# One attention kernel's first forty microseconds: the first pair's key rows sent in halves ahead of the second pair's key loads, and the second pair's turning moved into the first score slots

## The chip, the cores and the metric

The kernel runs on one core of one Trainium2 chip. The metric is device microseconds (us) of one execution; a time quoted without more is the median of several runs. Lower is better.

## The reference

The inputs are `q`, `k`, `v` of shape (2, 8, 768, 64), a projection of shape (64, 6), and the weights of two expert layers. Only the first part matters here:

```python
q_bits = (np.einsum('bhsd,dk->bhsk', q, proj) > 0)
k_bits = (np.einsum('bhsd,dk->bhsk', k, proj) > 0)
q_bucket, k_bucket = np.sum(q_bits * powers, -1), np.sum(k_bits * powers, -1)
mask = q_bucket[:, :, :, None] == k_bucket[:, :, None, :]
scores = np.where(mask, scale * q @ k.T, -1e9)      # per head
attn = exp(scores - max); attn /= sum(attn) + 1e-9
attn_out = attn @ v
x = moe(attn_out)      # dense: h = x w_in, a rational function of h, times w_out
out = moe2(x)          # each token to the expert with the largest logit
```

A query may only see keys whose six projection signs equal its own. Sixteen heads of 768 rows go through this, then 1536 tokens through a dense layer and through eight experts.

## The kernel before

Heads are taken in eight **pairs**; the two heads of a pair lie side by side in the 128 partitions (64 channels each). Each float32 matrix is split into a rounded high part and a rest (`qk_hi`, `qk_lo`), so that matmuls of rounded operands keep the precision. For each head an **operand** tile of four planes is built. Plane 0 and plane 1 are the stationary side of the score matmuls (high and low query rows; high query rows and query mask words). Plane 2 and plane 3 are the moving side (key rows twice; low key rows and key mask words). Two matmuls per bank then give score plus mask penalty at once.

**Preparing a pair** takes ten steps, `step(p, k)`, with one PSUM bank (number 7) between them. Steps 0 to 3 turn the loaded rows: three transposes on TensorE (PE), and an eviction to `raw` by ScalarE (ACT, steps 0 and 2, queries) or VectorE (DVE, steps 1 and 3, keys). GpSimd (POOL) then splits each half into `qk_hi` and `qk_lo` (`split_qk`). Steps 4 and 7 are six projection matmuls whose signs ACT writes to `bits`; steps 5, 6, 8 and 9 are one matmul each, whose mask words DVE writes. Each step waits until the one before it has been evicted. Rows that must change partition go by DMA from SyncE's queue (SP): `operand_rows`, `mask_rows`.

**The first pair** has a faster path of its own. It is loaded in halves of three tiles, turned into banks 0 to 3, and split straight out of PSUM by ACT (`first_split`: `qk_hi`) and DVE (`qk_lo`). PE projects the halves (`first_proj_hi`, `first_proj_lo`), ACT takes the signs, PE multiplies by `sel` (`first_sel`), and DVE (`first_mask`) and ACT (`first_word`) write the mask words. POOL copies the rows of head 0 that stay in their partitions (`first_own`), and SP sends the rows that change partition.

**The order of work** is written out by hand, in slots numbered `s`. Every second slot starts a score tile `scores(g)` (4 matmuls, `g = s/2`), which waits for `exp_done >= g - 1`, since two score tiles share the banks. DVE takes the row maximum (`maxs`), ACT the exponential (`exps`). From slot 7 PE turns the exponentials in chunks (`turn(c)`), ACT and DVE split them (`hi(c)`, `lo(c)`), and from slot 10 PE multiplies them by the values (`pv(j)`). `PREP_AT_1` names the slots after which the ten steps of the second pair stand: 3, 6, 7, 8, 9, ... 14. The third pair's first step is at slot 15. `keep_warm(n, bank)` is n matmuls of 512 columns on zeros, to no use but to keep PE going: 9 before the first load has landed, 3 ahead of slot 0, and 3 in each of slots 3, 4 and 6.

**SP's queue** at the start: the identity, the first pair's queries, two blocks of constants, then head 0 of the second pair (queries and keys), the first half of the low query rows (after `first_lo` 1), the second head's queries, the key rows of both halves in one transfer (after `first_hi` 4), the second half of the low query rows (after `first_lo` 3), the second head's keys, the values, and the rows of head 1.

Of the kernel before, what the change touches and what calls it, by code (L numbers as in the profile page):

```python
# [15 lines left out]
P = 128  # L16
B, H, S, D = 2, 8, 768, 64
NBITS = 6
# [97 lines left out]
def build(nc, q, k, v, proj, w_in, w_out, a, b, w_gate, w1, w2, consts, out):  # L116
    ctx = ExitStack()
    M4 = QF // P
    with ctx:
# [189 lines left out]
        s_half = sem("s_half")  # L309
        s_qk = [sem(f"s_qk{i}") for i in range(2)]  # L310
        s_v = [sem(f"s_v{i}") for i in range(2)]
        s_op = [[sem(f"s_op{i}{o}") for o in range(2)] for i in range(2)]
# [136 lines left out]
        PREP_AT = [1, 2, 3, 4, 8, 9, 10, 12, 13, 14]  # L449
        PREP_AT_1 = [3, 6, 7, 8, 9, 10, 11, 12, 13, 14]  # L450
        PREP_AHEAD = 10
# [69 lines left out]
        def op_landed(p, o):  # L521

            return 96 * (p // 2 + 1) - (0 if p % 2 else (64, 16)[o])

# [39 lines left out]
        def _(sp):  # L564
# [66 lines left out]
            sp.dma_start(cst[:, P:C_END], consts[:, P:C_END]).then_inc(s_const, 16)  # L631
            load_qk_head(1, 0, 0)
            load_qk_head(1, 0, 1)
            sp.wait_ge(first_lo, 1)
            sp.dma_start(operands[0][0][D:P, 0, 0:HALF].bitcast(F32), qk_lo[0][0:D, 0, 0:HALF].bitcast(F32)).then_inc(s_op[0][0], 16)
            load_qk_head(1, 1, 0)
            sp.wait_ge(first_hi, 4)
            sp.dma_start(operands[0][0][D:P, 2, :].bitcast(F32), qk_hi[0][0:D, 1, :].bitcast(F32)).then_inc(s_op[0][0], 16)
            sp.wait_ge(first_lo, 3)
            sp.dma_start(operands[0][0][D:P, 0, HALF:S].bitcast(F32), qk_lo[0][0:D, 0, HALF:S].bitcast(F32)).then_inc(s_late_lo, 16)  # L640
            load_qk_head(1, 1, 1)
            load_v(0)
# [83 lines left out]
        def _(pool):  # L726
# [52 lines left out]
            pool.wait_ge(first_lo, 4)  # L779
            pool.tensor_copy(operands[0][0][0:D, 3, :], qk_lo[0][0:D, 1, :].bitcast(F32)).then_inc(first_own, 1)  # L780
            split_v(0)
            split_qk(1, 0)
            split_qk(1, 1)
# [92 lines left out]
        def _(act):  # L876
# [9 lines left out]

            act.wait_ge(s_proj, 32)
            act.wait_ge(zeroed, 2)
            for x in range(4):
                rows = slice(x % 2 * D, (x % 2 + 1) * D)  # L890
                act.activation(wproj[rows, x // 2 * 2, x * NBITS:(x + 1) * NBITS], pr_raw[rows, :], ACT.Copy).then_inc(proj_hi, 1)
            first_split(0)
# [8 lines left out]
            def first_word(half, o):  # L901
# [4 lines left out]
                               scale=BIG, bias=cst[other, C_CUT:C_CUT + 1]).then_inc(first_high, 1)  # L906

            first_word(1, 0)
            first_word(0, 1)
            first_word(1, 1)  # L910
# [222 lines left out]
        def _(dve):  # L1133
# [5 lines left out]
            def first_split(half):  # L1139

                for x in range(2):
                    k, c = 2 * half + x, slice(half * HALF, (half + 1) * HALF)
                    dve.wait_ge(first_hi, k + 1)
                    dve.scalar_tensor_tensor(out=qk_lo[0][:, x, c], in0=ps[:, k, 0:HALF], scalar=(0.125, 1.0)[x], in1=qk_hi[0][:, x, c].bitcast(F32), op0=ALU.mult, op1=ALU.subtract).then_inc(first_lo, 1)

            dve.wait_ge(proj_hi, 4)
            for x in range(4):
# [21 lines left out]
            def step(p, k):  # L1169
# [5 lines left out]
                if k in (1, 3):  # L1175
                    dve.wait_ge(prep_pe, m + 1)
                    if k == 1 and p >= 2:
                        for o in range(2):
                            dve.wait_ge(s_op[p % 2][o], op_landed(p - 2, o))
                    dve.tensor_copy(raw[p % 2][:, 1, c], bank).then_inc(prep_out, 1)  # L1180
                elif k in (5, 8):
                    dve.wait_ge(prep_pe, m + 1)
                    if k == 5:
                        for o in range(2):
                            dve.wait_ge(s_op[(p - 1) % 2][o], op_landed(p - 1, o))
                    dve.tensor_scalar(mask[:, 0, c], bank, NBITS - 0.5, BIG, ALU.is_ge, ALU.mult).then_inc(prep_out, 1)
                elif k in (6, 9):
                    dve.wait_ge(prep_pe, m + 1)
                    dve.tensor_scalar(mask[:, 1, c], bank, -float(NBITS), -1.0, ALU.add, ALU.max).then_inc(prep_out, 1)
# [280 lines left out]
        def _(pe):  # L1470
            def step(p, k):
# [6 lines left out]
                if m == 0:  # L1478
                    pe.wait_ge(first_dve, 1)
                    pe.wait_ge(first_high, 2)  # L1480
                if k < 4:
                    pe.wait_ge(s_qk[p % 2], 64 * (p // 2 + 1))
                    for t in range(HT):
# [23 lines left out]
            def scores(g):  # L1507
# [4 lines left out]
                if g == 0:  # L1512
                    pe.wait_ge(first_own, 3)
                    pe.wait_ge(first_dve, 3)
                    pe.wait_ge(first_high, 1)
                if g == HT:
                    pe.wait_ge(s_late_lo, 16)
                if g == NT:
                    pe.wait_ge(first_dve, 5)
                    pe.wait_ge(first_high, 3)  # L1520
# [95 lines left out]
            first_sel(1)  # L1616
            keep_warm(3, 3)

            for s in range(NSLOT):
# [15 lines left out]
                if prep_at(s):  # L1635
                    step(*prep_at(s))
                if s == 3:
                    pe.wait_ge(first_dve, 4)
                if s in (3, 4, 6):
                    keep_warm(3, 6)  # L1640
                r = turn_r_at(s)
# [328 lines left out]
```

## Time and profile before

| | us |
|---|---|
| median of 3 runs | 802.01 (801.35 to 804.67) |
| profiled execution, its own time | 802.68 |
| profiled execution, span from first to last instruction | 800.8 |
| PE busy in the span | 782.6 |
| DVE, ACT, POOL busy | 563.2, 498.6, 457.8 |

Busy time counts work, not the issue of DMAs. PE's busy time includes the matmuls on zeros, and the modelled end of a matmul overlaps the next one, so the distance between two starts is the better price of a matmul than its duration. PE is the LDWEIGHTS and MATMUL engine; PEld is its weight load alone; SPq is SyncE's queue issuing a DMA.

### The profile page before, as it was taken

The page shows a single profiled execution, that of the slowest core. Times are in us where ns is not written, and L with a number is a line of the kernel's source. Part 1 is how long each engine was busy: PE and PEld are TensorE (multiplying, and loading weights), DVE is VectorE, ACT ScalarE, POOL GpSimd, SP SyncE. Part 2 cuts the span into 40 slices and gives each one's busy share as a digit, 9 for nine tenths or more (in the row PEclk, how much of TensorE's full clock was granted, in tenths as well). Part 3 has the DMA queues.
Part 4 walks back from the last instruction along what each step waited for, and adds up shares of the span by engine and source line. Part 5 has one row for each costly group of instructions (what it writes and reads, how often), then busy time and mean ns, then how long its engine had stood idle before and what let it go on. Part 6 is the DMA issues. An engine that isn't in the chain of part 4 may idle for free.

```text
span 800.8 us, 13465 instructions
## 1 busy us (share of the span) xinstructions
PE 782.6 (98%) x4305; PEld 692.0 (86%) x4305; DVE 563.2 (70%) x973; ACT 498.6 (62%) x988; POOL 457.8 (57%) x405
## 2 busy tenths in 40 slices
PE   8899999999999999999999999999899999999997
PEld 6799899899998989999999999997688888888886
DVE  5788888888887787887778877997354454444542
ACT  5688878878898998778778877874332224222100
POOL 3425265265257687457647744533997659755810
PEclk9999999999999999999999999997999999999999
DMA  8899977985841760950692041063664447433200
GB/s 194 171 215 199 211 164 168 204 169 132 191 150 53 237 244 0 338 203 1 204 374 83 1 156 55 3 206 125 210 234 151 181 146 254 155 132 132 68 33 19
DMA packets 71986, 123.49 MB, mean 154 GB/s; under 512 B 33358, under 2 KB 36270, under 8 KB 67824
## 3 DMA queue, kind: packets, MB, share of 16 engines
q1 hardware_dynamic: 64320, 90.77, 41.9%
q10 hardware_dynamic: 5056, 25.56, 8.9%
q0 software_dynamic: 2544, 6.31, 2.2%
q8 instruction: 37, 0.61, 0.3%
q14 instruction: 29, 0.24, 0.1%
HBM read 60.33 MB, written 34.24 MB: 118 GB/s over the span
## 4 chain that ended last, share of the span: by engine, by line
PE 90%; ACT 3%; issue 2%; DVE 2%; DMA 1%; POOL 0%; POOLq 0%; SPq 0%; ACTq 0%; DVEq 0%
PE ps L1538 7%; PE ps L1574 6%; PE ps L1576 6%; PE ps L1575 6%; PE ps L1675 5%; PE ps L1676 5%; PE ps L1674 5%; PE ps L1872 4%; PE ps L1904 4%; PE ps L1902 4%; PE ps L1903 4%; PE ps L1873 4%; PE ps L1877 4%; PE ps L1525 4%; PE ps L1550 4%; PE ps L1526 4%
## 5 line engine op out<-in xcount | busy, mean ns | idle before, releaser
L841 POOL TENSOR_TENSOR split<-wraw,split 128x512 f32 (+1 forms) x112 | 140.5, 1296 | 46.3 <-ACT split L1031 42.1
L1031 ACT ACTIVATE split<-wraw 128x512 f32 (+1 forms) x128 | 69.4, 619 | 120.3 <-PE ps L1904 56.2
L1215 DVE TENSOR_TENSOR ptl<-ps,pth 128x512 fp32r<-128x512 f32 x144 | 98.8, 686 | 37.2 <-ACT pth L945 35.3
L945 ACT ACTIVATE pth<-ps 128x512 fp32r<-128x512 f32 x144 | 86.5, 601 | 32.9 <-PE ps L1538 32.8
L816 POOL TENSOR_TENSOR hw<-hw,ha 128x384 f32<-128x384 f32 x64 | 65.3, 1020 | 72.3 <-ACT hw L981 72.3
L1195 DVE TENSOR_REDUCE negmax<-ps 128x1 f32<-128x768 f32 x96 | 91.0, 949 | 8.5 <-PE ps L1526 8.5
L936 ACT ACTIVATE pr<-ps,negmax 128x768 f32<-128x768 f32 x96 | 86.8, 904 | 4.2 <-DVE negmax L1195 4.2
L1538 PE MATMUL ps<-cst,pr 128*128 128x128 f32 x576 | 88.0, 273 | 1.2 <-ACT pr L936 1.2
L1574 PE MATMUL ps<-xh,wih 128*128 128x384 f32 x256 | 86.6, 338 | 0.0
L1576 PE MATMUL ps<-xh,wil 128*128 128x384 f32 x256 | 86.3, 337 | 0.0
L1575 PE MATMUL ps<-xl,wih 128*128 128x384 f32 x256 | 85.9, 336 | 0.0
L551 POOL TENSOR_TENSOR gl<-ha,gh 128x384 fp32r<-128x384 f32 x64 | 65.0, 1016 | 27.7 <-ACT gh L545 27.7
L1538 PEld LDWEIGHTS ps<-cst,pr 128*128 128x128 f32 x576 | 69.8, 140 | 8.6 <-ACT pr L936 2.2
L1550 PE MATMUL ps<-pth,vs 128*128 128x384 f32 x192 | 74.3, 387 | 0.2
L1525 PE MATMUL ps<-operand 128*128 128x384 f32 x192 | 68.8, 358 | 1.2 <-DMA operand<-qk_hi 0.7
L1676 PE MATMUL ps<-woh,gl 128*128 128x512 f32 x168 | 66.5, 396 | 0.0
L1675 PE MATMUL ps<-wol,gh 128*128 128x512 f32 x168 | 66.4, 395 | 0.0
L1674 PE MATMUL ps<-woh,gh 128*128 128x512 f32 x168 | 65.4, 389 | 0.0
L1551 PE MATMUL ps<-ptl,vs 128*128 128x384 f32 x192 | 64.9, 338 | 0.0
L1526 PE MATMUL ps<-operand 128*128 128x384 f32 x192 | 64.6, 337 | 0.0
L1443 DVE TENSOR_SCALAR yo<-ps,gi 128x512 f32<-128x512 f32 x18 | 13.5, 750 | 68.1 <-PE ps L1904 68.1
L1902 PE MATMUL ps<-split,hth 128*128 (+1 forms) x144 | 57.7, 401 | 1.1 <-DVE htl L1434 1.1
(240 smaller groups left out, 2018.7 us busy)
## 6 DMA issues: line engine op xcount, KB each, us to landing
routed<-blank SPq DMA_DIRECT2D x33, 771.0 KB, 13.6
wraw<-in_moe_w ACTq DMA_DIRECT2D x24, 1024.0 KB, 6.5
wraw<-in_moe_w SPq DMA_DIRECT2D x8, 1024.0 KB, 6.2
operand<-qk_hi SPq DMA_DIRECT2D x31, 192.0 KB, 4.6
operand<-qk_hi SPq DMA_DIRECT2D x15, 384.0 KB, 4.9
operand<-qk_lo SPq DMA_DIRECT2D x30, 192.0 KB, 4.3
operand<-mask SPq DMA_DIRECT2D x14, 384.0 KB, 5.2
xg<-routed SPq DMA_DIRECT2D x19, 256.0 KB, 2.7
```

Source lines behind the costliest of these rows:

```text
L841: pool.tensor_tensor(split_piece(E_LO[x], ring, k), wraw[:, x, i, :], split_piece(E_HI[x], ring, k).bitcast(F32), ALU.subtract).then_inc(e ...
L1215: dve.tensor_tensor(ptl[:, at:at + CW], ps[:, 4 + c % 2, :], pth[:, at:at + CW].bitcast(F32), ALU.subtract).then_inc(ptl_done, 1)
L1525: pe.matmul(bank, operand_of(n, 0)[:, rows], operand_of(n, 2)[:, cols], start=True, stop=False)
L1526: mm = pe.matmul(bank, operand_of(n, 1)[:, rows], operand_of(n, 3)[:, cols], start=False, stop=True)
L1538: mm = pe.transpose(ps[:, 4 + c % 2, x * P:(x + 1) * P], pr[u % UNITS][:, t, kt * P:(kt + 1) * P], ident)
L1550: pe.matmul(ps[:, 6, 0:HALF], vs[n % 2][:, kt, :], pth[:, cols], start=(kt == 0), stop=False)
L1574: pe.matmul(bank, wh[:, kt, f], xh[bb][:, kt, cols], start=(kt == 0), stop=False)
L1575: pe.matmul(bank, wh[:, kt, f], xl[bb][:, kt, cols], start=False, stop=False)
L1576: mm = pe.matmul(bank, wl[:, kt, f], xh[bb][:, kt, cols], start=False, stop=(kt == KD - 1))
L1674: pe.matmul(ps[:, 4 + t, :], gh[s % 2][:, m, rows], woh[qq % 2][:, m, :], start=(m == 0), stop=False)
L1675: pe.matmul(ps[:, 4 + t, :], gh[s % 2][:, m, rows], wol[qq % 2][:, m, :], start=False, stop=False)
L1676: mm = pe.matmul(ps[:, 4 + t, :], gl[s % 2][:, m, rows], woh[qq % 2][:, m, :], start=False, stop=(m == M4 - 1))
```

## The change

1. SP loads both heads' queries of the second pair ahead of everything that waits, under a semaphore of their own (`s_second_q`). The key rows of head 0 go in two halves, the first as soon as `first_hi` is 2. Both key loads of the second pair stand behind them, and the second half of the low query rows behind those.
2. The copies that make the high part of `wproj` move from ACT to DVE.
3. ACT's mask words come in another order (head 1's first half first). `scores(0)` no longer waits for `first_high`; `scores(3)` does.
4. Step 0 of the second pair stands ahead of slot 0, the other steps at slots 2, 4, 6, 8, 9, 10, 11, 12 and 13. The matmuls on zeros fall from 3 to 1 ahead of slot 0, and from 9 to 3 inside the slots (2 in slot 2, 1 in slot 6).
5. POOL splits the second pair's first half before it splits head 0's values. The mask step of the second pair no longer waits for head rows of the first.

```diff
-        PREP_AT_1 = [3, 6, 7, 8, 9, 10, 11, 12, 13, 14]
+        PREP_AT_1 = [-1, 2, 4, 6, 8, 9, 10, 11, 12, 13]
...
-            return 96 * (p // 2 + 1) - (0 if p % 2 else (64, 16)[o])
+            return 96 * (p // 2 + 1) - (0 if p % 2 else (48, 16)[o])
...
-            load_qk_head(1, 0, 0)
-            load_qk_head(1, 0, 1)
+            for o in range(2):
+                sp.dma_start(nat[1][:, 0, :, o, :], q_h[2 + o, :, :, :]).then_inc(s_second_q, 16)
+
+            def first_rows(x, plane, rows, half, landed):
+
+                c = slice(half * HALF, (half + 1) * HALF)
+                sp.dma_start(operands[0][0][D:P, plane, c].bitcast(F32), rows[0:D, x, c].bitcast(F32)).then_inc(landed, 16)
+
+            sp.wait_ge(first_hi, 2)
+            first_rows(1, 2, qk_hi[0], 0, s_op[0][0])
             sp.wait_ge(first_lo, 1)
-            sp.dma_start(operands[0][0][D:P, 0, 0:HALF].bitcast(F32), qk_lo[0][0:D, 0, 0:HALF].bitcast(F32)).then_inc(s_op[0][0], 16)
-            load_qk_head(1, 1, 0)
+            first_rows(0, 0, qk_lo[0], 0, s_op[0][0])
             sp.wait_ge(first_hi, 4)
-            sp.dma_start(operands[0][0][D:P, 2, :].bitcast(F32), qk_hi[0][0:D, 1, :].bitcast(F32)).then_inc(s_op[0][0], 16)
+            first_rows(1, 2, qk_hi[0], 1, s_op[0][0])
+            for o in range(2):
+                load_qk_head(1, o, 1)
             sp.wait_ge(first_lo, 3)
-            sp.dma_start(operands[0][0][D:P, 0, HALF:S].bitcast(F32), qk_lo[0][0:D, 0, HALF:S].bitcast(F32)).then_inc(s_late_lo, 16)
-            load_qk_head(1, 1, 1)
+            first_rows(0, 0, qk_lo[0], 1, s_late_lo)
...
+            split_qk(1, 0)
             split_v(0)
-            split_qk(1, 0)
...
-            act.wait_ge(s_proj, 32)
-            act.wait_ge(zeroed, 2)
-            for x in range(4):
-                rows = slice(x % 2 * D, (x % 2 + 1) * D)
-                act.activation(wproj[rows, x // 2 * 2, x * NBITS:(x + 1) * NBITS], pr_raw[rows, :], ACT.Copy).then_inc(proj_hi, 1)
...
+            first_word(0, 1)
             first_word(1, 0)
-            first_word(0, 1)
...
+            dve.wait_ge(s_proj, 32)
+            dve.wait_ge(zeroed, 2)
+            for x in range(4):
+                rows, cols = slice(x % 2 * D, (x % 2 + 1) * D), slice(x * NBITS, (x + 1) * NBITS)
+                dve.tensor_copy(wproj[rows, x // 2 * 2, cols], pr_raw[rows, :]).then_inc(proj_hi, 1)
...
-                    if k == 5:
+                    if k == 5 and p >= 2:
...
-                    pe.wait_ge(first_high, 2)
+                    pe.wait_ge(first_high, 1)
                 if k < 4:
-                    pe.wait_ge(s_qk[p % 2], 64 * (p // 2 + 1))
+                    if p == 1 and k % 2 == 0:
+                        pe.wait_ge(s_second_q, 32)
+                    else:
+                        pe.wait_ge(s_qk[p % 2], 64 * (p // 2 + 1) - (32 if p % 2 else 0))
...
-                    pe.wait_ge(first_high, 1)
                 if g == HT:
                     pe.wait_ge(s_late_lo, 16)
+                    pe.wait_ge(first_high, 2)
...
-            keep_warm(3, 3)
+            step(1, 0)
+            keep_warm(1, 3)
...
-                if s == 3:
+                if s == 2:
                     pe.wait_ge(first_dve, 4)
-                if s in (3, 4, 6):
-                    keep_warm(3, 6)
+                if s in (2, 6):
+                    keep_warm((2, 1)[s // 6], 6)
```

## Rows read from the trace of the kernel before

**Rows 1.** The page: busy time, share of the span and instructions

```profile
PE 782.6 (98%) x4305; PEld 692.0 (86%) x4305; DVE 563.2 (70%) x973; ACT 498.6 (62%) x988; POOL 457.8 (57%) x405
```

**Rows 2.** Windows: from:to, length, busy us of each engine, granted clock, DMA share, GB/s

```profile
8.00:13.00 5.00, 3.93 (x20) 2.65 (x20) 3.96 (x9) 3.76 (x8) 3.00 (x3) 1.00 0.75 163
...
40.00:50.00 10.00, 10.00 (x66) 9.43 (x65) 8.22 (x13) 7.80 (x16) 4.48 (x5) 1.00 0.99 215
```

**Rows 3.** PE's waits from 0 to 60 us: total, times, longest

```profile
PE ps L1489 <- DVE raw L1180: 0.7, 1, 0.7
...
PE ps L1484 <- DVE raw L1180: 0.4, 1, 0.4
```

**Rows 4.** Timeline of the start: start, us, what, idle before and its releaser

```profile
5.48 2.49 PE L1587 MATMUL ps<-cst,nat 128*128 128x128 f32 x12
5.79 0.90 ACT L891 ACTIVATE wproj<-pr_raw 64x6 fp32r<-64x6 f32 x4 [1.55 <-DMA pr_raw<-in_proj]
6.71 1.85 ACT L885 ACTIVATE qk_hi<-ps 128x384 fp32r<-128x384 f32 x4
6.71 0.73 DVE L1149 TENSOR_TENSOR wproj<-pr_raw,wproj 64x6 fp32r<-64x6 f32 x4 [4.60 <-ACT wproj L891]
...
8.56 0.19 PEld L1600 LDWEIGHTS ps<-qk_lo,wproj 128*128 128x128 f32 x1 [0.20 <-DVE qk_lo L1144]
...
10.43 0.82 POOL L780 CAST operand<-qk_lo 64x768 fp32r<-64x768 f32 x1
...
10.92 2.12 DVE L1161 TENSOR_SCALAR operand<-ps 64x384 fp32r<-64x384 f32 x4
11.27 1.65 ACT L905 ACTIVATE operand<-ps,cst 64x384 fp32r<-64x384 f32 x3 [0.43 <-PE ps L1607]
...
12.83 0.44 PE L1525 MATMUL ps<-operand 128*128 128x384 f32 x1 [0.74 <-DMA operand<-qk_hi]
```

**Rows 5.** DMA issues by kind, 0 to 13 us: KB each, us to landing

```profile
operand<-qk_lo SPq DMA_DIRECT2D x2, 96.0 KB, 2.8
operand<-qk_hi SPq DMA_DIRECT2D x1, 192.0 KB, 3.5
```

**Rows 6.** Groups of one shape, 0 to 60 us: busy us, mean ns, idle before

```profile
L1195 DVE TENSOR_REDUCE negmax<-ps 128x1 f32<-128x768 f32 x18 | 17.0, 951 | 5.1 <-PE ps L1526 5.1
L1215 DVE TENSOR_TENSOR ptl<-ps,pth 128x512 fp32r<-128x512 f32 x21 | 14.4, 685 | 6.4 <-ACT pth L945 6.1
...
L936 ACT ACTIVATE pr<-ps,negmax 128x768 f32<-128x768 f32 x17 | 15.3, 901 | 3.0 <-DVE negmax L1195 3.0
L945 ACT ACTIVATE pth<-ps 128x512 fp32r<-128x512 f32 x21 | 12.6, 598 | 8.0 <-PE ps L1538 8.0
...
L735 POOL TENSOR_TENSOR qk_lo<-raw,qk_hi 128x768 fp32r<-128x768 f32 x4 | 7.3, 1834 | 0.3
```

**Rows 7.** The chain that ended last: start, us on the chain, what

```profile
16.91 0.70 PE ps L1556 x3
...
18.31 0.33 PE ps L1484 x3
```

**Rows 8.** Timeline of PE later: start, us, what, idle before

```profile
15.94 0.44 PE L1525 MATMUL ps<-operand 128*128 128x384 f32 x1 [0.43 <-ACT pr L936]
...
27.15 0.41 PE L1525 MATMUL ps<-operand 128*128 128x384 f32 x1
...
33.63 0.55 PE L1484 MATMUL ps<-cst,nat 128*128 128x128 f32 x3 [0.55 <-DVE mask L1189]
...
37.84 0.42 PE L1525 MATMUL ps<-operand 128*128 128x384 f32 x1
```

**Rows 9.** DMA issues by kind, 0 to 40 us

```profile
nat<-in_k SPq DMA_DIRECT2D x4, 192.0 KB, 3.9
```

**Rows 10.** Timeline and windows about 545 us

```profile
543.48 1.91 PE L1699 MATMUL ps<-wg,yt 128*128 128x8 f32 x16
...
545.00:550.00 5.00, 4.79 (x19) 3.59 (x19) 3.86 (x21) 4.14 (x9) 1.60 (x2) 0.68 0.28 86
```

More of the change, by code:

```diff
@@ L310, in build @@
         s_qk = [sem(f"s_qk{i}") for i in range(2)]
+        s_second_q = sem("s_second_q")
         s_v = [sem(f"s_v{i}") for i in range(2)]
```

## The prediction

> **What bounds the kernel now.** I read the page first. PE is busy 782.6 of 800.8 us [rows 1], so only 18.2 us are to be had at all without taking real work from it, and the change takes away no real work: it touches the first forty microseconds and leaves the rest alone. The windows come next. From 40 to 50 us PE is busy for all 10.00 us [rows 2]; from there on what PE has gained earlier it keeps, and it can gain no more. So the question is how much earlier PE reaches that steady stretch. For this I read PE's waits from 0 to 60 us and then the timeline. The reader is to see four waits for the work this change moves: 0.7 us of a projection for an eviction of the second pair and 0.4 us for another eviction [rows 3], 0.74 us for the key rows' transfer ahead of `scores(0)` [rows 4], and 0.55 us of the third pair's first transposes for the last mask words of the second, shown with the later rows. Beside them lie the matmuls on zeros, which count as busy and are none: twelve from slot 0's front to slot 6.
>
> **What the start gains.** `scores(0)` starts at 12.83 us, behind the key rows, which took 3.5 us to land and so left at 9.3 [rows 4, 5]. This is one transfer of 192 KB behind a load of the second pair that was issued just before it.
>
> After the change the first transfer is due when ACT's second `qk_hi` piece is there. ACT loses its four copies to `wproj` (5.79 to 6.69), but PE's transposes run from 5.48 to 7.97, and the last of ACT's four pieces begins at 6.71 + 3 x 1.85 / 4 = 8.1 already, 0.1 behind the last transpose [rows 4]. So the first two pieces come up to 0.3 earlier, the last two at the old time, 8.56. The last half of the key rows is then issued at about 8.7, the queue being free, and its 96 KB land after the 2.8 us of such pieces [rows 5], at 11.5, at the latest after the 3.5 of today's 192 KB, at 12.2.
>
> DVE makes the copies ACT made. The trace has no such copy on DVE; the nearest row is its subtraction of the same shape, 0.73 / 4 = 0.18 each with its gap [rows 4]. As bounds I take that and half of it: the low part of `wproj` is done at 5.79 + 8 x 0.18 = 7.2, or at 6.9. DVE's first `qk_lo` piece can start at 7.2 instead of just after 6.71 + 0.73 = 7.44. PE takes 0.2 of this, its idle time before L1600 [rows 4]; the rest is bound by its own transposes. So the signs, the mask matmuls and the mask words come 0.2 earlier. `scores(0)` waits for the third mask piece of DVE: today 10.92 and two of the four pieces of 2.12, so 12.0 [rows 4], then 11.8. This is the later of the two, and ahead of it PE fits step 0 (three transposes, 0.35, from 11.3, when ACT's first mask word has freed the bank; ACT's words start when `bits` is written, 0.4 ahead of today's 11.27) and one matmul on zeros, to 11.9. POOL's own copies are done at 10.43 + 0.82 = 11.25 [rows 4] and stay so. **`scores(0)` starts at 11.9 instead of 12.83: 0.9 us**, and the cause of waiting is now DVE, no longer a transfer.
>
> **What the slots gain.** I walk on with the durations of the rows: maximum 0.95, exponential 0.90 and 0.1 until its sum is read, high part 0.60, low part 0.69, POOL's low part 1.83 [rows 6], copy and mask 0.55 (2.12 / 4 and a little [rows 4]). PE's prices are distances on the chain: three transposes 0.33, so four 0.45, and a matmul of 512 columns 0.70 / 3 = 0.23 [rows 7], so 0.175 for 384 columns: 0.70 for a score tile, 1.05 for six projection matmuls, 0.35 for two of `pv`.
>
> The first tiles are a chain: score, maximum, exponential, next score but one. It is 15.94 - 12.83 = 3.1 us long [rows 4, 8], so `scores(2)` is at 15.0. Steps 1 and 2 lie inside this chain's idle time. Step 1 wants the key loads: issued at about 9.4 and 10.0, 3.9 us to landing [rows 9], so 13.9; needed, with two matmuls on zeros behind, by 14.2. This is the nearest thing to a new wait, and 0.3 is all that covers it. `scores(3)` follows at 16.05 and needs the second half of the low query rows, issued at 10.65: at 3.5 us it is there at 14.2. The exponential of tile 2 ends at 18.05, `turn(0)` starts then, `scores(4)` at 18.6. Today the steps 1, 2 and 3 each sit here with an eviction in between. After the change only their last eviction is open, and PE goes through `turn(1)`, step 4 and `turn(2)` to 21.25, waits 0.4 for the signs, and has `scores(5)` at 21.85. POOL's first split (a copy of under 0.9 and the low part, 2.7 together) is ready at 15.5 + 2.7 = 18.2, its second at 22.6, both ahead of their projections; the values are split by 19.9, needed at 22.5.
>
> Now part is given back. The mask steps come in consecutive slots, and DVE has a maximum and a low part to do between two of them: PE waits 0.25 before step 6, 0.5 before step 7, 0.75 before step 9. `scores(6)` comes at 26.05 against 27.15 [rows 8]: the lead is down to 1.1. But all ten steps are over one slot earlier, and the third pair's first step finds its bank free: it starts at 31.0, where today it starts at 33.63 after a wait for that mask [rows 8]. Three more evictions (ACT at 33.3, DVE at 35.15) lead to `scores(9)` at 35.5 against 37.84 [rows 8].
>
> **The sum: 37.84 - 35.5 = 2.3 us**, of which 0.9 is the start. As a cross-check: the eight matmuls on zeros that go are worth 1.9 at 0.23 each if nothing takes their place, and the four waits are 2.4 [rows 3, 4, 8]; the walk keeps 2.3 of these 4.3. The bounds are 0.9 (all behind the start given back) and 4.3.
>
> The copies on DVE are hidden by PE's transposes; without that cover they would cost 0.7. SP's queue issues as many transfers up to the values as before, so these and head 1's rows leave at today's times; the second pair's rows leave earlier, when POOL is done at 22.6. The dropped wait of the mask step costs and gives nothing: those rows were long sent.
>
> The profiled execution took 802.68 with a span of 800.8, so the sum gives a span of 798.5 and 800.4 in all; against the median of 802.0 I put **799.7**.
>
> **Rivals.** *Given back.* DVE's queue between mask steps is the new bound; should each of the six waits of the walk be 0.2 longer than its idle time today, the lead at `scores(9)` is 2.3 - 1.2 = 1.1: 800.9. For it speaks that DVE waits for ACT's high part 6.1 us already, more than for PE's scores [rows 6]; against it, that PE's end of the steps is moved a whole slot.
>
> *The start is not moved.* ACT loads its function table ahead of its first piece of work, today while it waits for the projection. If that now falls behind its wait for PE, its pieces come later and the start's gain is gone: 2.3 - 0.9 = 1.4, 800.6. If instead the key loads or the low rows behind them land over 1 us later than in their rows, step 1 or `scores(3)` takes up the start's gain, with the same result, and a second such us brings it to 801.6.
>
> *More.* If DVE's order fits better than in my walk, its three mask waits vanish (1.5 us): 3.8 in all, 798.2. And if the clock's fall further down (next rival) does not come, or comes where it costs less, up to half of its length is won beside any of these: the shift of all later work may decide that, and its sign is open.
>
> *The other side: the clock.* Eight matmuls on zeros go, where PE already has gaps. In this trace the clock fell once, between 545 and 550 us, where its mean is 0.68: part at full, part at the lower of its two levels, 1.2 GHz [rows 10]. PE was busy 4.79 of these 5 us; just before, it had done short work, 16 matmuls of 8 columns. If that came between 13 and 23.5 us, the walk's 7.9 us of PE work there would take twice as long, less the 2.3 us of idle time it fills: 5.6 more, 805.3. It decides from the point at which about half of that stretch is low. Against it: from 8 to 13 us PE was busy 3.93 of 5 us only, and the clock stood at 1.00 [rows 2]. The Trainium skill (TensorE: Matmul & The Clock Gate, Part 1) says that the throttled state is the default and activity releases it, so it speaks against taking filler matmuls away; taken alone it would give the 805.3. This trace's fall agrees in kind, its start so far does not.
>
> **How the numbers follow.** The forecast (798.9 to 800.5) has 0.47. Given back 0.20, start not moved or the loads late 0.15, more 0.13, clock 0.05. Eight in ten lie between 797.7 and 801.8, which leaves out the clock and the far end of each other case. Half a per cent is 4.0 us, about what a measurement of this kernel can tell from no change; the forecast lies inside it. Faster than 798.0 needs "more" and a little beyond, 0.10; slower than 806.0 needs the clock and a mishap, 0.02; 0.88 is left for the same.
>
> **What the changed profile would show.** Right: the first score matmul at 11.9 waiting for DVE or nothing; PE's wait for the transfer gone; third pair's first transposes near 31 without a wait for a mask; DVE mask or `bits` waits of 0.3 to 0.7 between 21 and 30; from 40 us on each score tile 2.3 earlier. Wrong: a wait of the first or fourth score tile or of step 1 for a DMA, a table load between PE's transposes and ACT's first piece, `scores(9)` within 1 us of 37.84, or a clock under 1.00 before 30 us.

## The result, and the profile after

| | before | changed |
|---|---|---|
| median of 5 runs (lowest to highest) | 802.01 (801.35 to 804.67) | 797.85 (797.26 to 799.17) |
| profiled execution, its own time | 802.68 | 797.85 |
| profiled execution, span | 800.8 | 795.7 |
| mean granted clock of the profiled execution | 0.993 | 0.995 |

The kernel before has two more runs here than in its own table; its median is the same. The ratio is 0.9945, 95% interval 0.9929 to 0.9962: faster by 0.5%, 4.2 us, where 2.3 were forecast and "the same" had 0.88. The interval reaches from 3.0 to 5.7 us, so that by these runs alone the change may lie on either side of half a per cent. The time is in the wide range (797.7 to 801.8), at its faster end, and outside the narrow one (798.9 to 800.5). More runs (below) put the changed kernel at 0.9958 (0.9941 to 0.9974).

The page of the changed kernel has eight matmuls fewer than [rows 1] and PE 4.2 us less busy:

```profile
PE 778.4 (98%) x4297; PEld 689.0 (87%) x4297; DVE 563.9 (71%) x977; ACT 497.6 (63%) x984; POOL 457.5 (57%) x405
```

The windows that answer to [rows 2] (columns as there):

```profile
8.00:13.00 5.00, 4.66 (x26) 3.42 (x25) 3.81 (x9) 3.89 (x9) 3.01 (x3) 1.00 0.83 176
...
40.00:50.00 10.00, 9.76 (x65) 8.70 (x64) 7.29 (x12) 7.36 (x16) 1.52 (x2) 1.00 1.06 228
```

The clock is 1.00 in both, with 4.66 instead of 3.93 us of work in the first. PE's waits from 0 to 60 us, which answer to [rows 3] (engine, tile, line, what it waited for: total, times, longest):

```profile
PE ps L1510 <- DVE mask L1195: 0.6, 1, 0.6
PE ps L1510 <- ACT bits L930: 0.5, 2, 0.2
PE ps L1496 <- DVE raw L1189: 0.4, 1, 0.4
...
PE ps L1496 <- DMA nat<-in_k: 0.3, 1, 0.3
PE ps L1501 <- DVE mask L1198: 0.2, 1, 0.2
```

The wait for the key rows and the one of 0.7 for an eviction are gone. Mask waits of 0.6 and 0.2 stand where the kernel before had two of 0.6 and 0.3; a second one of 0.2 for the signs (`bits`) is new, and so is one of 0.3 in step 1, for a key load. The timeline of the start and of PE's later score tiles answers to [rows 4] and [rows 8]:

```profile
11.89 0.41 PE L1537 MATMUL ps<-operand 128*128 128x384 f32 x1
...
13.80 0.52 PE L1496 MATMUL ps<-cst,nat 128*128 128x128 f32 x3 [0.26 <-DMA nat<-in_k]
...
14.98 0.44 PE L1537 MATMUL ps<-operand 128*128 128x384 f32 x1 [0.19 <-ACT pr L940]
...
18.03 0.44 PE L1550 MATMUL ps<-cst,pr 128*128 128x128 f32 x2 [0.17 <-ACT pr L940]
...
18.22 0.42 PE L1537 MATMUL ps<-operand 128*128 128x384 f32 x1
...
21.37 0.47 PE L1537 MATMUL ps<-operand 128*128 128x384 f32 x1
...
24.34 0.44 PE L1501 MATMUL ps<-qk_hi,wproj 128*128 128x384 f32 x1 [0.20 <-DVE mask L1198]
...
25.48 0.33 PE L1537 MATMUL ps<-operand 128*128 128x384 f32 x1
...
28.66 0.34 PE L1510 MATMUL ps<-bits,sel 128*128 128x384 bf16 x1 [0.56 <-DVE mask L1195]
...
30.32 0.49 PE L1496 MATMUL ps<-cst,nat 128*128 128x128 f32 x3
...
34.17 0.55 PE L1496 MATMUL ps<-cst,nat 128*128 128x128 f32 x3 [0.40 <-DVE raw L1189]
34.48 0.42 PE L1537 MATMUL ps<-operand 128*128 128x384 f32 x1
```

`scores(0)` starts at 11.89 as forecast, the third pair's first transposes wait for nothing, and `scores(9)` comes at 34.48 against 37.84 in [rows 8]: 3.36 us earlier, not 2.3.

To follow this lead further I compare the start of the same instruction in both traces. DVE's maximum of score tile 20, before and then changed:

```profile
65.67 0.95 DVE L1195 TENSOR_REDUCE negmax<-ps 128x1 f32<-128x768 f32 x1
```

```profile
62.28 0.95 DVE L1204 TENSOR_REDUCE negmax<-ps 128x1 f32<-128x768 f32 x1
```

The lead is 3.39. It is 3.40 at the last score tile (252.15 and 248.75), so nothing is lost or won in 190 us. Then, in the router and at the first expert's output, before:

```profile
543.75 0.67 DVE L1320 TENSOR_SCALAR pick<-iota,slotf 128x128 fp32r<-128x128 f32 x3
...
579.21 0.74 DVE L1443 TENSOR_SCALAR yo<-ps,gi 128x512 f32<-128x512 f32 x1
```

and changed:

```profile
540.30 0.67 DVE L1329 TENSOR_SCALAR pick<-iota,slotf 128x128 fp32r<-128x128 f32 x3
...
574.25 0.74 DVE L1452 TENSOR_SCALAR yo<-ps,gi 128x512 f32<-128x512 f32 x1
```

3.45 at the first, 4.96 at the second. Between the two the granted clock differs. The windows before (the column ahead of the last two is the granted clock; the window of 545 to 550 is in [rows 10]):

```profile
540.00:545.00 5.00, 4.95 (x40) 4.71 (x41) 4.22 (x20) 1.94 (x4) 1.07 (x2) 1.00 0.54 149
...
550.00:555.00 5.00, 5.00 (x21) 3.36 (x20) 2.85 (x13) 1.56 (x4) 2.74 (x4) 0.50 0.38 146
555.00:560.00 5.00, 5.00 (x24) 3.36 (x23) 3.45 (x12) 1.35 (x3) 1.43 (x2) 0.79 0.36 139
```

and changed:

```profile
540.00:545.00 5.00, 5.00 (x29) 4.61 (x29) 4.08 (x18) 3.20 (x8) 0.14 (x1) 0.68 0.22 58
545.00:550.00 5.00, 4.72 (x21) 3.37 (x22) 2.67 (x15) 1.83 (x4) 2.75 (x3) 0.64 0.41 158
550.00:555.00 5.00, 4.78 (x25) 3.11 (x25) 4.51 (x20) 2.67 (x5) 2.88 (x3) 1.00 0.41 160
```

With two levels, 1.2 and 2.4 GHz, a mean of 0.68 over 5 us is 3.2 us at the lower. Before, with the first window of the fall in [rows 10], that makes 3.2 + 5.0 + 2.1 = 10.3 us; changed 3.2 + 3.6 = 6.8. These 3.5 us less at half the clock are worth up to 1.75 us of matmuls, enough for the 1.5.

So the span's difference of 5.1 us has two parts: about 3.4 made in the first forty microseconds, and about 1.5 that fit a fall of the clock that was shorter in this execution. Whether the second part belongs to the change is a question for many executions.

### The profile page after: what moved, and what is told of

Same layout as the page of the kernel before. It is cut to its first block, busy times and chain, and to the rows that moved or that the text cites. A ratio compares the mean times of both kernels' runs of the same rounds, so it can differ in the third digit from the quotient of the medians.

```text
span 795.7 us, 13448 instructions
## 1 busy us (share of the span) xinstructions
PE 778.4 (98%) x4297; PEld 689.0 (87%) x4297; DVE 563.9 (71%) x977; ACT 497.6 (63%) x984; POOL 457.5 (57%) x405
## 3 DMA queue, kind: packets, MB, share of 16 engines
q0 software_dynamic: 2544, 6.31, 2.2%
## 4 chain that ended last, share of the span: by engine, by line
PE 90%; ACT 4%; issue 2%; DVE 2%; DMA 1%; SPq 0%; POOLq 0%; POOL 0%; ACTq 0%; DVEq 0%
PE ps L1550 7%; PE ps L1586 6%; PE ps L1588 6%; PE ps L1587 6%; PE ps L1688 5%; PE ps L1689 5%; PE ps L1687 5%; PE ps L1915 4%; PE ps L1917 4%; PE ps L1916 4%; PE ps L1885 4%; PE ps L1886 4%; PE ps L1890 4%; PE ps L1537 4%; PE ps L1538 4%; PE ps L1562 4%
## 5 line engine op out<-in xcount | busy, mean ns | idle before, releaser
L1433 DVE TENSOR_SCALAR hs<-ps 128x512 f32<-128x512 f32 x38 | 26.3, 691 | 46.5 <-PE ps L1890 43.7
```

## Theories and experiments

**A**, that of the prediction: the start gives 0.9, the rest comes of all ten steps standing earlier, so that the last step is out of the third pair's way. **B**: the second pair's first four steps, three transposes each, now stand where the first tiles leave PE idle, and the last six matter little. **C**: the matmuls on zeros alone had cost what is won, and taking them away is the gain. **D**: the halves of the key rows are what gives the start. **E**: the late fall of the clock draws its length anew in each execution, and the change has no part in it. "Lead" below is the start of tile 20's maximum, 65.67 before, less that of the experiment; it repeats within 0.13 us between two executions of the changed kernel (62.28 and 62.41), so one profile tells large differences, while times need many runs. It has limits. The kernel before has one trace only. The first score matmul starts between 11.89 and 12.18 in seven executions whose program is the same up to there (the changed kernel, e5, e8, e11, e12, e14, e15). And in some variants the lead moves by up to 0.4 between tile 43 and tile 90. Leads that differ by less than 0.3 or so are not told apart.

Times are compared in a second way too. Most of their scatter goes with the mean granted clock of the execution (shown under e5), so each run's time is brought to a clock of 0.994 at 0.53 us per 0.001 and the mean taken: the **time at equal clock**, known to 0.2 to 0.4 us with six to ten runs. It is 801.93 for the kernel before.

**e1. The old kernel with the new number of zeros.**

```diff
-            keep_warm(3, 3)
+            keep_warm(1, 3)
...
-                if s in (3, 4, 6):
-                    keep_warm(3, 6)
+                if s in (3, 6):
+                    keep_warm((2, 1)[s // 6], 6)
```

> The kernel before with the matmuls on zeros alone cut as in the change (1 ahead of slot 0, 2 in slot 3, 1 in slot 6, instead of 3, 3, 3 and 3). The measure is the start of DVE's maximum of score tile 20: 65.67 us before, 62.28 changed, so 3.39 earlier. Theory A (early slots are bound by chains over DVE and ACT, and most zeros lie in idle time of PE): 0.4 to 0.9 us earlier. Rival B (the zeros are PE work like any other): eight times 0.23, 1.9 us earlier.

Tile 20 at 66.25: a lead of -0.58, neither A's 0.4 to 0.9 nor B's 1.9. Median 801.54 (10 runs) against 802.36 (31 of before on the same chip), ratio 0.9990 (0.9978 to 1.0002); at equal clock 801.5, 0.4 faster. The lead does not isolate the zeros: 0.25 us of it were gone at `scores(0)`, whose transfer landed later, and the clock fell behind that. But C falls by the times, and by e2 and e3 below, which had no such fall. The timeline shows the clock rival of the prediction, in the old kernel:

```profile
13.08 0.44 PE L1525 MATMUL ps<-operand 128*128 128x384 f32 x1 [1.56 <-DMA operand<-qk_hi]
...
13.73 0.53 PE L1526 MATMUL ps<-operand 128*128 128x384 f32 x1
14.05 0.53 PE L1525 MATMUL ps<-operand 128*128 128x384 f32 x1
```

and its windows:

```profile
8.00:13.00 5.00, 3.18 (x17) 2.14 (x16) 3.89 (x8) 3.72 (x8) 3.00 (x3) 1.00 0.78 163
13.00:18.00 5.00, 4.92 (x19) 4.45 (x20) 2.06 (x3) 2.36 (x5) 0.83 (x2) 0.66 1.08 242
```

PE waited 1.56 us, and soon after the score matmuls went from a distance of 0.175 us to 0.32, for 3.4 us. The wait alone does not bring this: in e10 (below) PE waited 1.82 us in the window from 13 to 18 and was busy for 3.18 of its 5 us, in e9 it was busy for 3.56 of the 5 us from 8 to 13 and waited 1.36 us until 13.25, and the granted clock stayed at 1.00 in both. What made the difference is open.

**e2 and e3. The changed kernel with the old slots**, with all twelve zeros (e2) and with four (e3). The edit is that of e2, without its zeros in slots 3, 4 and 6; e3 keeps `keep_warm(1, 3)` and the four zeros of the changed kernel.

```diff
-        PREP_AT_1 = [-1, 2, 4, 6, 8, 9, 10, 11, 12, 13]
+        PREP_AT_1 = [3, 6, 7, 8, 9, 10, 11, 12, 13, 14]
...
-            step(1, 0)
-            keep_warm(1, 3)
+            keep_warm(3, 3)
```

> The changed kernel with all ten steps of the second pair at the old slots and all twelve matmuls on zeros: the new start alone. Theory A: the maximum of tile 0 starts 0.9 us earlier than before (13.91), and that of tile 20 0.9 to 1.1 earlier. Rival C (the start's lead is lost behind the evictions of the steps, so all of the gain is the slots'): tile 20 under 0.3 earlier.

> The changed kernel with the steps at the old slots and only four matmuls on zeros: new start and fewer zeros, no new slots. Theory A: tile 20 is 1.3 to 2.0 us earlier than before, and the rest to 3.39 is the placement of the steps. Rival B (start and zeros are all of it): 2.8 to 3.4 earlier.

e2: lead 1.11, 800.54 (10 runs), ratio 0.9981 (0.9966 to 0.9995), at equal clock 800.9. e3: lead 1.35, 801.32 (10), ratio 0.9986 (0.9972 to 1.0001), at equal clock 800.7; from tile 44 on its lead is 1.1 too. The start is worth 1.1, and in the old slots the zeros are worth at most 0.25. The start here is all of the change but slots and zeros: ACT's new order of mask words, POOL's earlier split of the second pair and the dropped wait are in it, and none of the three was run alone. Whether the new slots need POOL's earlier split is not shown.

**e4. No zeros at all; e6, all of them** (three ahead of slot 0, three each in slots 2, 4 and 6), both in the changed kernel.

```diff
-            keep_warm(1, 3)
...
-                if s in (2, 6):
-                    keep_warm((2, 1)[s // 6], 6)
```

> The changed kernel without its last four matmuls on zeros. Theory A: the granted clock stays at 1.00 from 8 to 60 us, and tile 20 starts within 0.3 us of 62.28, earlier if at all. Rival D (the zeros hold the clock): the granted clock falls between 10 and 30 us, and tile 20 starts over 2 us later.

> The changed kernel with twelve matmuls on zeros again: 3 ahead of slot 0 and 3 in each of slots 2, 4 and 6. Theory A (they fit idle time only in part, and each beyond that is in the chain): tile 20 starts 0.5 to 1.2 us later than 62.28. Rival B (PE work like any other): 1.9 later. Rival G (all of it idle time): within 0.2.

e4: lead 3.09, at the far edge of A's 0.3; 799.59 (10), ratio 0.9959 (0.9944 to 0.9975), at equal clock 798.6. The clock did not fall:

```profile
13.00:18.00 5.00, 3.83 (x24) 2.86 (x22) 4.00 (x5) 3.15 (x6) 2.44 (x2) 1.00 1.04 229
```

e6: lead 2.24, 799.46 (10), ratio 0.9966 (0.9952 to 0.9980), at equal clock 799.4. In the new order eight more zeros cost 3.39 - 2.24 = 1.15 us of tile 20, by e5's profile 1.02, by the times 0.8; less than their 1.9. The cut is needed for part of the gain, but is not its source.

**e5. The changed kernel again**, ten runs.

> The changed kernel as it is, run many times more. So far its five runs had a mean clock of 0.9954 and the runs of the kernel before 0.9929; in those the time moves by 0.56 us for each 0.001 of clock. Theory E (the walk's part is 3.4 us, the rest of the 4.2 was a better draw of the late fall of the clock): the mean clock comes out within 0.001 of the kernel before and the median near 799.0, 3.4 below it; the maximum of tile 20 starts between 62.1 and 62.6. Rival F (the change itself shortens the fall): the mean clock stays at 0.995 or over and the median near 798.

Lead 3.26, 799.22 (796.27 to 801.52), ratio 0.9958 (0.9941 to 0.9974), 24 runs of before. Within 31 runs of before, time and mean granted clock have a correlation of -0.96. Fitted over all 83 runs of before and all 15 of the changed kernel, the time at a mean clock of 0.994 is 801.93 and 798.60, with slopes of 0.53 and 0.50 us per 0.001: **3.3 us apart at equal clock**, the lead of the trace. The mean clocks are 0.9930 and 0.9939; the difference, 0.0009, is worth 0.5 us, and 15 runs cannot tell it from none. The first five runs had 0.995, 0.997, 0.997, 0.995 and 0.993, a mean of 0.9954; e5's ten, of the same kernel, 0.9932. So E holds: the first five drew well.

**e7. The key rows in one transfer**, still ahead of the second pair's key loads.

```diff
-            return 96 * (p // 2 + 1) - (0 if p % 2 else (48, 16)[o])
+            return 96 * (p // 2 + 1) - (0 if p % 2 else (64, 16)[o])
...
-            sp.wait_ge(first_hi, 2)
-            first_rows(1, 2, qk_hi[0], 0, s_op[0][0])
...
-            first_rows(1, 2, qk_hi[0], 1, s_op[0][0])
+            sp.dma_start(operands[0][0][D:P, 2, :].bitcast(F32), qk_hi[0][0:D, 1, :].bitcast(F32)).then_inc(s_op[0][0], 16)
```

> The changed kernel with head 0's key rows in one transfer again, after the fourth high piece, still ahead of the key loads. Theory A (the start now waits for DVE's mask words, and the order in the queue is what counts, not the halves): the first score matmul starts within 0.3 us of 11.9. Rival H (192 KB take their 3.5 us wherever they stand): it starts at 12.1 to 12.3 waiting for the transfer. With the order of the queue undone as well it would be 12.8.

First score matmul at 11.96 without a wait for the transfer, which was issued at 8.44; lead 3.26; 799.11 (7 runs), ratio 0.9948 (0.9928 to 0.9968), at equal clock 798.5. D falls: the halves are worth nothing here, where DVE's mask words are ready no sooner (in e3 and e4, with less in front on PE, `scores(0)` waited for them until 11.85 and 12.07).

**e9. Both key loads ahead of the last half of the key rows** (one profile).

```diff
-            sp.wait_ge(first_hi, 4)
-            first_rows(1, 2, qk_hi[0], 1, s_op[0][0])
             for o in range(2):
                 load_qk_head(1, o, 1)
+            sp.wait_ge(first_hi, 4)
+            first_rows(1, 2, qk_hi[0], 1, s_op[0][0])
```

> The changed kernel with both key loads of the second pair ahead of the second half of the key rows in the queue. Theory A (the place in the queue is what the start gained): the last half leaves 1.3 us later, lands at 12.9 or later, and the first score matmul starts at 12.9 to 13.7 waiting for it. Rival K (DVE's mask words set the start anyway): 11.9 to 12.1.

```profile
13.25 0.44 PE L1537 MATMUL ps<-operand 128*128 128x384 f32 x1 [1.36 <-DMA operand<-qk_hi]
```

Lead 1.94, 1.3 to 1.5 less than the changed kernel's. The last half left at 9.69 instead of 8.46. With the key loads ahead of it the whole gain of the start is gone (13.25, where the kernel before had 12.83): the order in SP's queue is what gives it.

**e10 and e13. The copies to `wproj` on ACT again**: the same kernel, first one profile, then ten runs.

```diff
+            act.wait_ge(s_proj, 32)
+            act.wait_ge(zeroed, 2)
+            for x in range(4):
+                rows = slice(x % 2 * D, (x % 2 + 1) * D)
+                act.activation(wproj[rows, x // 2 * 2, x * NBITS:(x + 1) * NBITS], pr_raw[rows, :], ACT.Copy).then_inc(proj_hi, 1)
```

> The changed kernel with the four copies to wproj on ACT again. Theory A (the walk): the first score matmul starts 0.1 to 0.3 us later than in the changed kernel (11.9 to 12.0 in two executions), and so does the maximum of tile 20. Rival L (ACT freed early is worth more, since its pieces lead the chain): 0.5 or more.

> The kernel of e10 once more, since there a key load took 5.2 us to land and PE waited 1.8 us for it in step 1. If that was one execution's landing: the first score matmul again near 12.05, the loads land in under 4 us, and tile 20 starts 0.1 to 0.4 us later than in the changed kernel. If issuing them 0.5 us later is what makes them late: a wait of over 1 us in step 1 again and tile 20 at 63.3 or later.

e10's lead was 2.12, with a wait that no theory had:

```profile
15.53 0.52 PE L1496 MATMUL ps<-cst,nat 128*128 128x128 f32 x3 [1.82 <-DMA nat<-in_k]
```

e13's was 3.13 without that wait, `scores(0)` at 12.09; 799.65 (10), ratio 0.9960 (0.9943 to 0.9978), at equal clock 798.7. The DMA issues of the first 13 us, e10:

```profile
nat<-in_k SPq DMA_DIRECT2D x2, 192.0 KB, 4.2
```

and e13:

```profile
nat<-in_k SPq DMA_DIRECT2D x2, 192.0 KB, 3.5
```

The wait belonged to one execution, in which one of the two key loads took 5.2 us to land. The copies are worth 0.1 to 0.3 of lead at the most, which one trace does not tell from nothing, and 0.1 by the times. e10 would have misled if it had stood alone, though it shows how close the prediction's late loads are.

**e11, e14 and e15. Part of the slots** (e11 and e14 one profile, e15 ten runs).

```diff
-        PREP_AT_1 = [-1, 2, 4, 6, 8, 9, 10, 11, 12, 13]
+        PREP_AT_1 = [-1, 2, 4, 6, 8, 9, 10, 12, 13, 14]   # e11
+        PREP_AT_1 = [-1, 2, 7, 8, 9, 10, 11, 12, 13, 14]  # e14
+        PREP_AT_1 = [-1, 2, 4, 6, 9, 10, 11, 12, 13, 14]  # e15
```

> The changed kernel with the last three steps of the second pair at their old slots 12, 13 and 14 and the first seven at the new ones. Theory M (what pays in the new slots is that the last mask words are read a slot earlier, ahead of the third pair's first step): tile 20 starts 0.7 to 1.5 us later than 62.3. Rival N (what pays is that the first evictions lie in the idle time of the first score tiles): within 0.4 of it.

> The changed kernel with the first two steps of the second pair at their new places and the other eight one after another from slot 7 to slot 14. Theory N (what pays is that evictions lie in idle time of the first tiles): half of the placement's 2 us, tile 20 at 63.0 to 63.8. If the first two alone matter: 62.3 to 62.7. If they do not matter: 64.3, as with the old slots.

> The changed kernel with the first four steps (the turning) at their new places, and the projection and mask steps in slots 9 to 14. Theory N: all of the gain is there, tile 20 within 0.3 us of 62.4. Rival M' (it also pays to be done with the masks early): 0.7 us later or more.

| | slots | lead |
|---|---|---|
| e2 | all old (twelve zeros) | 1.11 |
| e3 | all old (four zeros) | 1.35 |
| e14 | the first two early | 1.00 |
| e15 | the first four early | 2.95 |
| e11 | all but the last three early | 3.16 |
| changed, e5 | all early | 3.39, 3.26 |

e15 leaves the last six steps at the very slots of the kernel before, and e14 the last eight. e15's time is 799.86 (10 runs), ratio 0.9964 (0.9949 to 0.9978). At equal clock e3 has 800.7, e15 798.7 and the changed kernel 798.6: the four turning steps bring 2.0 us, and the other six 0.1, which is within the error. In e11 the third pair's first step has its wait back:

```profile
30.47 0.55 PE L1496 MATMUL ps<-cst,nat 128*128 128x128 f32 x3 [0.56 <-DVE mask L1198]
```

and the lead hardly changes. A's second half falls and B stands: with the four turning steps early nearly all is there, with two of them nothing (e14 has one profile only, and started 0.3 late). Steps 2 and 3 are those whose evictions PE waited for between slots 7 and 9: 0.21 us ahead of step 3 and 0.69 ahead of step 4 in the kernel before, 0.32 and 0.69 in e3, 0.49 and 0.69 in e14. In e15 both waits are gone.

**e8. The mask words of steps 5, 6 and 8 ahead of the low part on DVE.**

```diff
-                if prep_at(s - 1):
-                    step(*prep_at(s - 1))
+                early = [x for x in (prep_at(s),) if x in ((1, 5), (1, 6), (1, 8))]
+                late = [x for x in (prep_at(s - 1),) if x and x not in ((1, 5), (1, 6), (1, 8))]
+                for x in late:
+                    step(*x)
...
+                for x in early:
+                    step(*x)
```

> The changed kernel with DVE writing the mask pieces of steps 5, 6 and 8 of the second pair ahead of the low part of the same slot, instead of after the next slot's maximum. Theory I (PE's waits of 0.36 and 0.72 us near 24 and 28 us are DVE's order): these waits go and tile 20 starts 0.5 to 1.0 us earlier than in the changed kernel. Rival J (the delayed low parts are what PE and ACT want next): within 0.2 of it, or later.

Lead 4.04, at the last score tile 3.63 (3.40 and 3.28 in the changed kernel's two profiles). The mask matmul that waited 0.56 waits no more; the other wait of Theory I, 0.20 ahead of step 7, stays:

```profile
27.90 0.34 PE L1514 MATMUL ps<-bits,sel 128*128 128x384 bf16 x1
```

798.58 (6 runs, 797.34 to 801.39), ratio 0.9948 (0.9931 to 0.9965), at equal clock 798.0, 0.6 under the changed kernel, give or take 0.4. DVE's queue was a bound of this stretch, as the prediction's "given back" had it, at the price of the walk and not above.

**e12. e8 with four matmuls of 384 columns on constants in the router**, after `turn_y(10)`, `turn_y(11)`, `logit(10)` and `logit(11)`, to no other use than to put longer work between the short.

```diff
+                    pe.matmul(ps[:, 4, 0:3 * P], cst[:, 0:P], cst[:, 0:3 * P], start=True, stop=True)
```

> The kernel e8_masks_first with four more useless matmuls of 384 unrounded columns, between the last short matmuls of the router near 540 us. Theory O (the late fall of the clock follows the short matmuls there, and its length is most of the spread between runs): the clock falls later or for less time, the mean clock rises by 0.002 or more, and the median drops by up to 1.5 us though the added matmuls cost up to 2.5. Rival P (the fall has another cause): the mean clock stays within 0.001 and the median rises by the 1 to 2.5 us that they cost.

The windows of e12. In every other profile of this study the second of them has a mean clock of 0.50 to 0.77:

```profile
540.00:545.00 5.00, 5.00 (x32) 4.02 (x30) 3.02 (x16) 2.00 (x5) 0.44 (x1) 1.00 0.23 57
545.00:550.00 5.00, 4.33 (x26) 2.82 (x26) 4.08 (x19) 3.37 (x7) 2.89 (x4) 1.00 0.41 158
...
560.00:565.00 5.00, 5.00 (x17) 4.09 (x18) 0.54 (x1) 0.00 (x0) 5.00 (x5) 0.66 0.35 111
```

Mean granted clock 0.9984 over five runs, against 0.9925 over e8's six, as Theory O had it. The times are 797.71 (797.61 to 798.93), ratio 0.9948 (0.9934 to 0.9962): the lowest median of the study and the narrowest spread, but hardly under e8's. At 0.53 us per 0.001 the clock should give 3.1. The added matmuls take most of it: in e12's trace the distances from each to the next work are 0.35, 0.65, 0.73 and 0.43, 2.2 in all. Clock and cost together come to 0.9 us, the difference of the two medians. That it beats the changed kernel by more than chance is not shown. Nor is it shown that the width of the added matmuls keeps the clock: more work of another shape in these places, or the shift that it brings, was not tried.

## Why the prediction was right or wrong

**The start: right.** 0.9 forecast, 0.94 between 12.83 and 11.89, with the transfer gone from the waits. Its reason was right in one half. The prediction had the last rows leave at 8.7, the queue being free, and land after the 2.8 us of a half; they left at 8.46. e7 and e9 show that the place in the queue carries the gain (1.36 us in e9), and the halves nothing, and e3 and e4 have `scores(0)` waiting for DVE's mask words, as forecast.

**Up to `scores(3)`: right**, 14.98 and 16.04 against 15.0 and 16.05.

**The step that failed is "The exponential of tile 2 ends at 18.05, `turn(0)` starts then, `scores(4)` at 18.6", and the length of the walk behind it.** Against the walk PE is earlier by:

| at | walk | measured | earlier by |
|---|---|---|---|
| `scores(4)` | 18.6 | 18.22 | 0.38 |
| `scores(5)` | 21.85 | 21.37 | 0.48 |
| `scores(6)` | 26.05 | 25.48 | 0.57 |
| third pair's first transposes | 31.0 | 30.32 | 0.68 |
| `scores(9)` | 35.5 | 34.48 | 1.02 |

The exponential did end then. `turn(0)` takes four transposes, of which only two need it; the other two went at 17.48, and at 18.03 these two alone are left, with the score tile 0.19 behind. The walk put all four there. It also had the price of four too high, 0.45, from three transposes on the chain. From start to start four cost 0.36, in the kernel before:

```profile
26.12 0.60 PE L1538 MATMUL ps<-cst,pr 128*128 128x128 f32 x4
...
26.48 0.42 PE L1550 MATMUL ps<-pth,vs 128*128 128x384 f32 x1
```

and in the changed one:

```profile
26.18 0.60 PE L1550 MATMUL ps<-cst,pr 128*128 128x128 f32 x4
26.54 0.42 PE L1562 MATMUL ps<-pth,vs 128*128 128x384 f32 x1
```

So of the 0.38 at `scores(4)`, 0.17 is the half of the chunk that was done, 0.09 the price, and 0.1 an addition that the trace does not have. Eight such chunks follow up to `scores(9)`. At 0.09 each they make up to 0.7, the size of the other 0.64; part of it lies under waits for other engines, so the exact split is not shown. Of the 0.64, 0.34 fell between the third pair's first step and `scores(9)`. The walk had 4.5 us there, with each of three evictions delaying the next step; the trace has 4.16 and one such wait, of 0.40, at 34.17. The kernel before has 4.21 for the same stretch (33.63 to 37.84 in [rows 8]), so the prediction's own rows had this part. Not one big error, then, but a walk that was always on the late side, and 1.0 of 3.36 us at its end.

**The mask waits: nearly right.** Forecast 0.25, 0.5 and 0.75. The rows show none, 0.20 and 0.56; between the starts of matmuls it is 0.11 (22.72 to 23.01, less 0.175), 0.36 and 0.72, since a modelled end lies 0.165 behind the next possible start. 1.2 instead of 1.5.

**"But all ten steps are over one slot earlier, and the third pair's first step finds its bank free": true, but not the cause.** The bank is free, at 30.32; in e11 it is not, and of the lead no more than 0.1 to 0.2 goes. Of the about 2.3 us that are not the start's, e15 keeps all but 0.3 to 0.4 by its lead and all but 0.1 by its times, and e14, with two turning steps early, none. The order is worth so much only with fewer zeros: with all of them 0.8 to 1.15 is lost (e6).

**The cross-check** had 4.3 to be had and trusted the walk's 2.3. The truth, 3.4, lies between. Two ways of counting that differ by 2.0 in a sum of 2.3 should have moved the forecast or widened it more than they did.

**The rivals.** "Given back": refuted for the size (e5), while e8 shows that DVE's queue costs 0.6 to 0.8 there, of which 0.2 to 0.35 is left at the last score tile. "Start not moved": the table load stayed where it was, at 2.90 us, long ahead of ACT's first piece at 6.31; `scores(0)` and `scores(3)` came as forecast in the changed kernel; in e10's execution a late load did come, and cost 1.0 of lead. The changed profile has one of the signs that the prediction had called wrong, a wait of step 1 for a DMA: 0.26 us at 13.80, with a key load that took 4.0 us to land. It cost nothing, as `scores(2)` behind it still waited 0.19 us for ACT. "More": its size nearly came (3.8 forecast, 3.4 measured), by another way than vanishing mask waits. The clock: it did not fall early in the changed kernel nor in e4 with no zeros at all, but it did in the old kernel with fewer zeros (e1), so the rival was real; the changed kernel escapes it in the profiles seen, and the runs do not tell by what. The prediction's "This trace's fall agrees in kind" is not borne out: the late fall came while PE counted as busy (4.95 of 5 us ahead of it, 4.79 in its first window). The late fall's sign was rightly left open: its length is drawn anew, 3.4 us in e5's profile, 6.8 in the first of the changed kernel, 13.7 in e7's, 17.1 in e8's.

**The verdict.** Of the first runs' 4.2 us, 3.3 to 3.4 belong to the change, and about 0.8 to those executions' clock. At 3.3 us, 0.4%, "the same" would have been right by the bound of 4.0; at 4.2 it was not. The mechanism missed by 1.0 us, and luck, the kind draw of the clock, added 0.8; either of them alone would have left the median inside the bound. The chance of 0.10 for "faster" left too little room for both together. The draw was named in the text; the error was not, since "more" counted on the mask waits alone.

## What to carry to other kernels

Look for filler work beside real work that waits elsewhere: real work moved into the filler's place brought 2.0 us here, taking the filler away alone at most 0.4. Price each chunk by its parts' own inputs, as half of a chunk may be ready before the chunk is, and hold each stretch of a walk against the same stretch of the trace that you have. And where the clock falls by chance in each execution, compare the kernels at equal mean clock, or by the start of one instruction ahead of the fall: here 3.3 at equal clock and 3.3 to 3.4 from one instruction, where the ratio of e5's ten runs has an interval of 1.3 us to either side. One profile does not tell differences under 0.3 us.

## What the runs showed of the hardware

- The late clock fall comes with PE busy, not after idle time: before, 4.95 of the 5 us ahead of it (540 to 545), 4.79 in its first window and 5.00 in the next. The Trainium skill (TensorE: Matmul & The Clock Gate, Part 1) ties the fast clock to activity; the rows here show a fall in a stretch that counts as busy but had short work just ahead ([rows 10]), and in e12, with wider matmuls there, none until 560. The fall in e1 followed a wait of 1.56 us; a wait of 1.82 us in e10 brought none.
- The same two loads of 192 KB landed in 3.5 us in one execution (e13) and in 4.2, the slower of them 5.2, in another (e10) of the same kernel: late enough for a wait of 1.82 us on PE.
- One transfer of 192 KB and two of 96 KB made no difference to the first score matmul (11.96 and 11.89), while two loads of 192 KB ahead in the queue made 1.36 us of waiting.
- The four copies to `wproj` took DVE 0.76 us in the changed trace, 0.19 each, its subtractions of the same shape 0.73: the first was no cheaper for having one operand.
